# A fused attention, top-2 experts and gated feed-forward kernel on one Trainium2 core: a new order on SyncE's queue in the expert stage, and expert weights loaded in pieces of 384 KB

## The reference

```python
for t in range(S):                                       # 1: gated linear attention
    state = f[:, :, t, :, None] * state + np.einsum('bhd,bhe->bhde', k[:, :, t], v[:, :, t])
    y[:, :, t] = np.einsum('bhd,bhde->bhe', q[:, :, t], state)
...
noisy_logits = logits + noise_scale * noise              # 2: router and top-2 of 8 experts
top2 = np.argpartition(-noisy_logits, 2, axis=1)[:, :2]
for e in range(E):
    for k in range(2):
        mask = top2[:, k] == e
        h = np.maximum(x[mask] @ w1[e], 0.0)             # 384 -> 1024
        out[mask] += top2_w[mask, k, None] * (h @ w2[e]) # 1024 -> 384
...
xn = x / rms * rms_g                                     # 3: norm, gated feed-forward 384 -> 1536 -> 384
g = xn @ w_gate
return (silu * val @ w_out).astype(np.float32)           # silu of g, val = xn @ w_val
```

## Time and profile before

| | us |
|---|---|
| median of three runs | 1313.16 |
| lowest, highest | 1310.71, 1314.28 |
| the profiled execution's own time | 1315.43 |
| its span, first to last instruction | 1314.0 |
| PE busy | 1214.7 (92%) |
| mean granted TensorE clock | 0.979 of full speed |

### The profile page before, as it was taken

One profiled execution on the slowest core, in us unless ns is written; L12 is line 12 of the kernel. 1 busy time (PEld: TensorE's weight loads), 2 busy tenths in 40 slices (PEclk: granted clock), 3 DMA queues, 4 the chain that ended last, 5 costly groups with the idle time before them and its releaser, 6 DMA issues.

```text
span 1314.0 us, 26299 instructions
## 1 busy us (share of the span) xinstructions
PE 1214.7 (92%) x8577; PEld 1118.2 (85%) x8578; DVE 682.3 (52%) x1274; ACT 495.5 (38%) x1033; POOL 445.0 (34%) x374
## 2 busy tenths in 40 slices
PE   4999999999999999999899889599999999999998
PEld 4777878778788888888798779499999999999997
DVE  7898888876243343434343334244444444444433
ACT  3666566653232232333333333232323323232321
POOL 8467777734662323232355440310110101010000
PEclk9999999999999999899899989799999999999999
DMA  5233333245456756565657564210110101010000
GB/s 213 90 99 123 128 126 119 65 161 223 160 173 228 236 179 229 177 228 176 231 174 237 189 218 141 84 37 19 37 32 24 55 3 53 18 36 18 0 19 19
DMA packets 93056, 156.87 MB, mean 119 GB/s; under 512 B 36912, under 2 KB 70960, under 8 KB 90544
## 3 DMA queue, kind: packets, MB, share of 16 engines
q1 hardware_dynamic: 84384, 107.81, 25.6%
q0 software_dynamic: 8592, 47.98, 10.5%
HBM read 103.52 MB, written 52.23 MB: 119 GB/s over the span
## 4 chain that ended last, share of the span: by engine, by line
PE 51%; DMA 15%; SPq 14%; issue 7%; POOL 6%; DVE 3%; ACT 2%; another core or an unknown queue 0%; DVEq 0%; POOLq 0%; ACTq 0%
DMA hid_rows<-hid 12%; PE pD L1957 12%; PE pA L1957 12%; PE pA L1971 8%; SPq L569 5%; SPq L556 5%; PE pA L1662 4%; PE pS L1971 4%; PE pA L1880 3%; PE pD L1851 2%; SPq L550 2%; SPq L574 1%; PE pS L1880 1%; POOL qk L639 1%; DVE W L1156 1%
## 5 line engine op out<-in xcount | busy, mean ns | idle before, releaser
L1851 PE MATMUL pD<-we,xsH 128*128 x612 | 189.9, 391 | 8.2 <-ACT hid L979 4.1
L1336 DVE STREAM_TRANSPOSE pA<-hidP 128x512 f32<-128x512 f32 x98 | 64.7, 705 | 232.8 <-DMA hidP<-hid_rows 232.8
L808 POOL DMA_INDIRECT pair<-y_sorted,y_row x48 | 46.2, 963 | 335.0 <-DVE z L1578 271.8
L1598 DVE TENSOR_TENSOR gs<-pD,sig 128x384 f32<-128x384 f32 x96 | 53.5, 558 | 192.2 <-ACT sig L1089 192.2
L1662 PE MATMUL pA<-W 64*128 64x128 f32 (+3 forms) x1920 | 137.8, 284 | 16.2 <-DVE W L1156 12.0
L1880 PE MATMUL pA<-we,hidH 128*128 (+1 forms) x464 | 126.9, 356 | 25.9 <-DVE hidL L1343 16.6
L1662 PEld LDWEIGHTS pA<-W 64*128 64x128 f32 (+3 forms) x1920 | 113.6, 171 | 35.6 <-DVE W L1156 18.6
L1851 PEld LDWEIGHTS pD<-we,xsH 128*128 128x128 f32 x612 | 113.9, 188 | 31.5 <-issue 9.7
L985 ACT ACTIVATE hidH<-pA 128x512 fp32r<-128x512 f32 x110 | 65.4, 599 | 189.7 <-DVE pA L1336 177.2
L1089 ACT ACTIVATE sig<-pD 128x384 f32<-128x384 f32 x96 | 47.2, 492 | 204.1 <-PE pA L1957 194.0
L1851 PE MATMUL pD<-we,xsL 128*128 x306 | 120.0, 392 | 0.0
(11 more groups left out here) (261 smaller groups left out, 2663.7 us busy)
## 6 DMA issues: line engine op xcount, KB each, us to landing
hid_rows<-hid SPq DMA_DIRECT2D x49, 512.0 KB, 2.7
hidP<-hid_rows SPq DMA_DIRECT2D x196, 128.0 KB, 2.8
stage<-w POOLq DMA_DIRECT2D x14, 1536.0 KB
qk<-qk_t SPq DMA_DIRECT2D x24, 512.0 KB, 3.6
y_sorted<-yo SPq DMA_DIRECT2D x55, 192.0 KB, 2.5
xs<-x_sorted SPq DMA_DIRECT2D x200, 48.0 KB, 1.8
fT<-f_t SPq DMA_DIRECT2D x12, 512.0 KB, 5.0
vN<-v_n SPq DMA_DIRECT2D x24, 256.0 KB, 2.8
```

What stands on the lines that cost most here:

```text
L1336: dve.transpose(pA[0][:, h].rearrange("p (k j t) -> p k j t", k=k, j=Q), hidP.rearrange("p (j k f) -> p k j f", j=Q, k=FC)[:, h * k:(h + 1 ...
L1598: dve.tensor_tensor(gs[:], pD[:, f % 2 * 512:f % 2 * 512 + TT], sig[f % 2][:], ALU.mult).then_inc(s_u, 1)
L1851: ins = pe.matmul(hidden_bank(t, h), (xsL if a else xsH)[t.par][:, k * P:(k + 1) * P], we[:, bass.ds(at + (b * WE + k * F + h * HF), HF)], ...
```

## The change: what it does

Two things are altered. On SP, the slot's order becomes: `store_rows(t-1)`, `store_hidden(t+2)`, `load_rows(t+4)`, `load_hidden(t+2)`. The load of a tile's activations now follows the store of the same tile in the same slot, with the four loads of x rows between. The start of the loop (slots 5 and 6) is written to match. On POOL, the weights of experts 2 to 7 and the three output matrices are loaded by `in_pieces`: DMAs of 768 columns (384 KB), each issued after the one before has landed. The eight pieces of an expert are issued one after the other inside `load_expert`, ahead of the splits of that expert. Experts 0 and 1 are loaded as before.

```diff
--- before.py
+++ after.py
@@ -40,6 +40,9 @@
 WE = KC * F
 OUT_A = (4 * WE - 2 * KC * F2) // DM
 assert WE == FC * DM
+PIECE = 768
+PIECES = WE // PIECE
+PIECES3 = KC * F2 // PIECE
 NL = len(LEVELS)
 FILLS = 1 + NL
 MASKED = 1 + len(SMALL)
@@ -590,17 +593,25 @@
             load_rows(Tile(8))
             store_hidden(Tile(5))
             load_hidden(Tile(5))
+            store_rows(Tile(4))
             store_hidden(Tile(6))
+            wait_alone(sp, s_tx, 6)
+            load_rows(Tile(9))
+            load_hidden(Tile(6))
 
             def slot(t):
-                if (t + 1).before(SLOTS) and not hidden_by_pe(t + 1):
-                    load_hidden(t + 1)
-                store_rows(t - 1)
-                if (t + 4).before(SLOTS):
-                    wait_alone(sp, s_tx, t.times(1, 1))
-                    load_rows(t + 4)
-                if (t + 2).before(SLOTS) and not hidden_by_pe(t + 2):
+                if t.c > FIRST_P or t.i is not None:
+                    store_rows(t - 1)
+                    if (t + 2).before(SLOTS) and not hidden_by_pe(t + 2):
+                        store_hidden(t + 2)
+                    if (t + 4).before(SLOTS):
+                        wait_alone(sp, s_tx, t.times(1, 1))
+                        load_rows(t + 4)
+                    if (t + 2).before(SLOTS) and not hidden_by_pe(t + 2):
+                        load_hidden(t + 2)
+                else:
                     store_hidden(t + 2)
+                    load_hidden(t + 2)
             slots(sp, slot)
             store_rows(Tile(SLOTS - 1))
 
@@ -744,10 +755,31 @@
                 pool.tensor_tensor(low, src, high.bitcast(F32), ALU.subtract).then_inc(s, 1)
             split.n = 0
 
+            def in_pieces(to, fr, s, at):
+
+                for n in range(fr.shape[-1] // PIECE):
+                    if n:
+                        pool.wait_ge(s, at + 16 * n)
+                    c = slice(n * PIECE, (n + 1) * PIECE)
+                    pool.dma_start(to[:, c], fr[:, c]).then_inc(s, 16)
+
+            def landed1(e):
+
+                return 16 + 16 * PIECES * (e - 1)
+
+            def landed3(n):
+
+                return landed1(E - 1) + 16 * PIECES3 * n
+
             def load_expert(e):
 
                 at = pool.value_load(turn_i[0:1, e:e + 1], min_val=0, max_val=E - 1)
                 pool.wait_ge(s_we, 2 * e)
+                if e > 1:
+                    in_pieces(stage1, w1[bass.ds(at, 1)].rearrange("a p c -> (a p) c"), s_stage1, landed1(e - 1))
+                    pool.wait_ge(s_stage1, landed1(e))
+                    in_pieces(stage2, w2[bass.ds(at, 1)].rearrange("a p c -> (a p) c"), s_stage2, landed1(e - 1))
+                    return
                 pool.dma_start(stage1[:], w1[bass.ds(at, 1)].rearrange("a p c -> (a p) c")).then_inc(s_stage1, 16)
                 pool.dma_start(stage2[:], w2[bass.ds(at, 1)].rearrange("a p c -> (a p) c")).then_inc(s_stage2, 16)
 
@@ -771,27 +803,27 @@
                     for s in s_sc:
                         pool.wait_ge(s, 64 * (NP // 4))
                 part = [we[:, (e % 2 * 4 + k) * WE:(e % 2 * 4 + k + 1) * WE] for k in range(4)]
-                pool.wait_ge(s_stage1, 16 * e)
+                pool.wait_ge(s_stage1, landed1(e))
                 if e > 1:
                     wait_alone(pool, s_g1, done1)
                 split(part[0], part[1], stage1[:], s_we)
-                pool.wait_ge(s_stage2, 16 * e)
+                pool.wait_ge(s_stage2, landed1(e))
                 if e > 1:
                     wait_alone(pool, s_g2, done2)
                 split(part[2], part[3], stage2[:], s_we)
             pool.wait_ge(s_we, 2 * E)
-            pool.dma_start(stage3[:], w_gate2).then_inc(s_stage1, 16)
-            pool.wait_ge(s_stage1, 16 * E)
+            in_pieces(stage3, w_gate2, s_stage1, landed3(0))
+            pool.wait_ge(s_stage1, landed3(1))
             split(gateH[:], gateL[:], stage3[:], s_last)
             pool.wait_ge(s_last, 1)
-            pool.dma_start(stage3[:], w_val2).then_inc(s_stage1, 16)
-            pool.wait_ge(s_stage1, 16 * (E + 1))
+            in_pieces(stage3, w_val2, s_stage1, landed3(1))
+            pool.wait_ge(s_stage1, landed3(2))
             done = pool.value_load(ends_i[0:1, E - 2:E - 1], min_val=1, max_val=SLOTS + 1)
             wait_alone(pool, s_g2, done)
             split(valH[:], valL[:], stage3[:], s_last)
             pool.wait_ge(s_last, 2)
-            pool.dma_start(stage3[:], w_out2).then_inc(s_stage1, 16)
-            pool.wait_ge(s_stage1, 16 * (E + 2))
+            in_pieces(stage3, w_out2, s_stage1, landed3(2))
+            pool.wait_ge(s_stage1, landed3(3))
             for high, c in ((outHa, slice(0, OUT_A * DM)), (outHb, slice(OUT_A * DM, F2C * DM))):
                 split(high[:], outL[:, c], stage3[:, c], s_last)
```

## The result

The changed kernel takes 1273.22 us (median of four runs, 1272.26 to 1279.08), the kernel before beside it 1313.72. The ratio is 0.9698, 95% interval 0.9657 to 0.9739. The forecast was 1265, its own range 1258 to 1269, the range for 8 in 10 1258 to 1287: the median is over the first and inside the second.

The account below looks back on a forecast made before the run. PE bounds the kernel, so only its idle and slow time can be won: 1315.4 - 41.2 - 12.3 = 1261.9, plus 3 and 2 left over, 1267; median 1265 us, own range 1258 to 1269, 8 in 10 1258 to 1287.

Parts of the forecast that it names:

- PE's waits and clock: Expert stage, 350 to 790 us: 41.2 us of PE's waits and 12.3 us of slowed clock would go.
- leftovers: Expert stage after the change: 3 us of waits at its start and 2 for odd waits under pieces.
- SP's slot: SP's queue: `load_hidden` starts 3.5 us after store, 3 to 4 everywhere, never 8; a slot takes 6.5 of 8.4 us.
- The new loop over the x rows: x loads queued behind ReLU wait: loop 7.45 of 8.37 us, costing nothing; as rival 1272 to 1280 us, chance 0.13.
- Its sign: For the x rows' loop: ACT's cast waits for `turn_x`, the ReLU for the cast, PE busy below 98%.
- a burst that costs 5.8 as before would be covered but for about 1.5 us: Activations' round trip on SP: its new slack leaves about 1.5 us, at `hid`, of a burst's 5.8 us.
- The period of a piece: POOL's 384 KB loads: issue 0.57, landing 2.8, 0.3 until the next instruction, 3.7 us together.
- gone at p = 4.2: End of POOL's chain: nine us left before the gathers at 3.7 us a piece, gone at 4.2.
- the rival's formula, 518 + 60p: When POOL ends, in us, if it never waits for PE, p being the period of a piece.
- the second rival's end: POOL becomes the bound at piece periods of 4.3 to 5.1 us: 1284 us at 4.6, 1308 at 5.0; chance 0.10.
- No parting of the traffic: DMA traffic: pieces don't part it, waits return as many small ones, 1295 to 1313 us; chance 0.03.
- slower: POOL as bound beyond a piece period of 5.2 us; at 5.9 it is 1357 us; chance 0.06.

Follow-up runs that it names:

- the kernels with one piece of each load: Only the first 384 KB of each load of experts 2 to 7 brought, matrices whole: 0.9622 of the kernel before with new order, 0.9738 with old.

## Why the prediction was right, and where it was off

**PE's waits and clock** (41.2 + 12.3 us) went as forecast: 3.0 are left, the clock is 1.00 from 350 to 742. For leftovers I had put 5 us; they are 3.0, both at the start of the stage.

**SP's slot.** `load_hidden` was to start 3.5 us after the store. In the changed kernel:

```profile
507.28 0.34 SPq L566 DMA_DIRECT2D hid_rows<-hid  x1
508.53 1.87 SPq L559 DMA_DIRECT2D xs<-x_sorted  x4
510.70 1.85 SPq L572 DMA_DIRECT2D hidP<-hid_rows  x4
```

It is 3.4, and the store follows the ReLU's end (506.48 + 0.60) by 0.2. The next store comes at 516.47, with SP waiting for the ReLU in between: it has room, as said. But the prediction had 3 to 4 us "everywhere", and that failed: in 11 of the 49 slots it is 4.3 to 7.1 us, with SP waiting for the store's landing. PE waits in none of these after 372 us, so the slack covers them; but under pieces the load of the activations can start 3.7 us later than its usual 3.4, more than the 1.4 that the prediction gave a piece.

**The new loop over the x rows** was named with its price and kept as a rival. Its sign is in the trace: DVE waits for `xs` 43 times, 105.1 us in all, and ACT for `turn_x` 133.4 us; in the kernel before it was 11.8 and 50.7. The order does it, not the pieces: with the new order alone DVE waits 128.2 us for `xs`.

```profile
ACT xsH L997 <- DVE pX L1360: 133.4, 46, 5.1
DVE pX L1360 <- DMA xs<-x_sorted: 105.1, 43, 4.2
```

PE is busy 389.0 of 392 us all the same, and the kernels with one piece of each load show that there is nothing to gain. Under pieces the rival is wrong. Under whole loads it decides (new order alone), and there my text was wrong: "a burst that costs 5.8 as before would be covered but for about 1.5 us" counted the activations' slack and forgot the x rows, whose slack the same edit had cut to 0.9.

**The period of a piece is the step that failed.** I had 3.7 us, from a line through two landings; the mean over the 60 periods of the chain is 4.58. From the start of the issue a piece takes 4.1 us to land (the median), and I had 0.57 + 2.8 = 3.4. The slope was near (0.00374 us per KB; 0.0036 to 0.0048 between 384 and 768 KB). The fixed part was not: 0.57 + 1.4 = 2.0 rested on a 192 KB gather behind the end of the stage, beside only the gathers around it, and it is 2.6 to 2.7 where the activations run beside it. The Trainium skill's fit (DMA: Bandwidth & Descriptors, the section on the anatomy of a SWDGE DMA) has 2.0 us fixed too, so the trace does not agree with it under this traffic. The Trainium skill's rule to batch to 1 MiB or more (same page, Bandwidth, under Measured) holds for the length of POOL's chain (41.9 us to spare at 1536 KB, none at 384) and fails for PE: 1536 KB at a time is the slowest of the sizes tried one at a time (0.9875).

**What the period cost.** Nine us were to be left at the end of POOL's chain, "gone at p = 4.2". At 4.58 POOL is the bound, and the rival's formula, 518 + 60p, gives 793. Less the 5.7 of the earlier start and 2.8 because the rest of an expert costs POOL 20.4 us and not 20.9, that is 785; the first gather is at 784.9. PE's wait before stage 3 is 13.2 us longer, and whole matrices or larger pieces give that back. So the forecast's sum was right for PE and 10.7 us low for the stretch (441.3; 479.1 - 53.5 + 5 = 430.6 was forecast). The profiled execution came out 5.3 over the sum (10.7 less 5.7 of the early start), the median 8.2 over. What happened is the forecast's gain with the second rival's end; I had given the latter 0.10. That the median is inside the range for 8 in 10 is no merit of the 3.7: by the rival's own reckoning the time at 4.58 would have been 1283, and the early start and the shorter rest of an expert took off 8.5 of that.

**No parting of the traffic, and slower**: neither is seen. The prediction set the Trainium skill's rule of turns between queues (the same page, Queues, rings and completion order) against the store of 8.6 us and found that the trace does not agree with an even share. That step does not follow: the rule is about packets, and an even share of packets is not one of bytes. The DMA queues of the kernel before in 512 to 526 us (POOL's is q0, SP's q1; packets, MB, share of the 16 engines):

```profile
q0 software_dynamic: 288, 3.15, 61.5%
q1 hardware_dynamic: 1254, 1.38, 32.6%
```

A packet of POOL's carries 10.9 KB, one of SP's 1.1, so by turns of packets too SP's transfers could be held up behind a burst; the trace neither shows nor refutes the rule. The pieces also make POOL's packets shorter (5.0 KB in 500 to 520 us of the changed kernel). That alone does not help: with the new order, pieces without the wait between them give 0.983 and whole loads 0.977.

## What to carry to other kernels

When bulk loads share the DMA engines with a latency-bound round trip, bound what is under way to the size whose landing fits in the slack, and not below: each piece pays its fixed landing again (2.6 to 2.7 us here), and an in-order engine that waits for pieces is a chain with a length of its own. Compute that chain to its end, with a landing time taken from under the same traffic, and compare it with what is queued behind it. When a reorder moves a load behind a store, give the moved load its own slack, and ask about it under the worst traffic as well as the usual.

## What I had not expected

A 384 KB load with nothing of its own queue ahead takes 4.1 us to land while 232 GB/s are moved in all, against 3.1 us from the issue's start for a 192 KB gather behind the end of the stage. Of the difference some 0.7 us are the size (192 KB at 0.0036 us).

Two loads of 1536 KB one after the other (0.9875) are worse than both at once (0.9765), with the new order in both. From the second of the six experts' loads on, PE has one wait for each in both kernels; that the delays of two neighbouring slots add up to a longer one is how I read the traces, and was not tried apart.
